# Diagonal term of four attention pairs in the weight stage: from three VectorE passes over row copies to one turned product and six narrow TensorE products

## The reference, cut to what matters

```python
for t in range(S):
    kt, vt, rt, wt = (k[:, :, t], v[:, :, t], r[:, :, t], w[:, :, t])
    cur = np.einsum('bhd,bhe->bhde', u[None] * kt, vt)
    y[:, :, t] = np.einsum('bhd,bhde->bhe', rt, state + cur)
    state = wt[:, :, :, None] * state + np.einsum('bhd,bhe->bhde', kt, vt)
...
a = x @ w1
b = x @ w2
h = a * b @ w3
return (h @ w_out)
```

## Time and profile before

| | us |
|---|---|
| median of 3 runs (lowest, highest) | 981.27 (980.72, 982.27) |
| time of the profiled execution | 980.96 |
| its span, first to last instruction | 979.2 |

### The profile page before, as it was taken

The page is one execution under the profiler, slowest core; times in us unless marked ns, Lnnn a source line. Parts: engine busy times, 40 slices in busy tenths (PEclk is TensorE's granted clock), DMA queues, the critical chain, the costliest instruction groups (busy, mean ns, idle before and its releaser), DMA issues.

```text
span 979.2 us, 18038 instructions
## 1 busy us (share of the span) xinstructions
PE 947.8 (97%) x6825; PEld 894.3 (91%) x6825; DVE 676.2 (69%) x1133; ACT 528.0 (54%) x986; POOL 222.8 (23%) x209
## 2 busy tenths in 40 slices
PE   6989999999999999999989999999999999999995
PEld 4656999999999999999989999999999999999995
DVE  6997769888888875437766765757767468565570
ACT  4454445454555544326545665756657467565560
POOL 0000000202020111021453233333243332334321
PEclk9999999999999999999999999999999999999998
DMA  9996343544445121126557887877968779787751
GB/s 346 302 320 184 115 142 116 160 150 129 134 143 163 50 71 38 51 67 234 188 161 191 237 278 233 250 235 220 307 205 247 254 207 292 218 242 256 200 156 17
DMA packets 94347, 183.74 MB, mean 188 GB/s; under 512 B 18274, under 2 KB 49764, under 8 KB 94260
## 3 DMA queue, kind: packets, MB, share of 16 engines
q1 hardware_dynamic: 80884, 161.90, 50.8%
q0 software_dynamic: 12976, 20.66, 10.2%
q10 hardware_dynamic: 400, 0.02, 0.0%
HBM read 156.94 MB, written 26.97 MB: 188 GB/s over the span
## 4 chain that ended last, share of the span: by engine, by line
PE 87%; DVE 5%; ACT 3%; issue 2%; DMA 1%; SPq 0%; another core or an unknown queue 0%; POOL 0%; DVEq 0%; ACTq 0%; POOLq 0%
PE pp L1231 20%; PE bank L1215 20%; PE bank L786 13%; PE bank L803 7%; PE fx L786 6%; PE fx L803 4%; PE yu L1274 3%; PE pp L184 3%; PE tr L1196 2%; PE yu L1256 1%; PE fx L1256 1%; PE yu L205 1%; PE yu L235 1%; PE tr L193 1%; DVE kdiv L263 1%
## 5 line engine op out<-in xcount | busy, mean ns | idle before, releaser
L1125 POOL DMA_INDIRECT result<-x2s,who x55 | 92.5, 1681 | 290.3 <-ACT x2s L1348 277.4
L1335 DVE SCALAR_TENSOR_TENSOR abl<-bank,abh 128x512 fp32r<-128x512 f32 x96 | 66.2, 691 | 113.7 <-ACT abh L1330 97.5
L976 POOL DMA_INDIRECT slot_entry<-entry,slot_i x48 | 52.1, 1086 | 334.7 <-DVE token_f L965 322.5
L1215 PE MATMUL bank<-xh,set_up_h 128*128 128x256 f32 x384 | 109.2, 284 | 0.0
L1215 PE MATMUL bank<-xh,set_up_l 128*128 128x256 f32 x384 | 108.6, 283 | 0.0
L1215 PE MATMUL bank<-xl,set_up_h 128*128 128x256 f32 x384 | 108.6, 283 | 0.0
L1330 ACT ACTIVATE abh<-bank 128x512 fp32r<-128x512 f32 x96 | 57.5, 599 | 85.1 <-PE bank L1215 79.6
L786 PE MATMUL bank<-xh,w12h 128*128 128x384 f32 x264 | 89.5, 339 | 1.0 <-DVE xl L483 0.9
L786 PE MATMUL bank<-xh,w12l 128*128 128x384 f32 x264 | 88.4, 335 | 0.0
L786 PE MATMUL bank<-xl,w12h 128*128 128x384 f32 x264 | 88.2, 334 | 0.0
L1231 PE MATMUL pp<-set_down_h,abh 128*128 128x384 f32 x256 | 87.7, 342 | 0.0
(11 more groups left out here) (254 smaller groups left out, 2641.4 us busy)
## 6 DMA issues: line engine op xcount, KB each, us to landing
up_raw<-in_moe_w SPq DMA_DIRECT2D x93, 512.0 KB
down_raw<-in_moe_w SPq DMA_DIRECT2D x124, 384.0 KB
wt<-in_w SPq DMA_DIRECT2D x16, 384.0 KB, 3.2
kt<-in_k SPq DMA_DIRECT2D x16, 384.0 KB, 3.1
rt<-in_r SPq DMA_DIRECT2D x16, 384.0 KB, 3.6
vs<-in_v_rows SPq DMA_DIRECT2D x16, 384.0 KB, 3.7
kn<-in_k_rows SPq DMA_DIRECT2D x16, 288.0 KB, 3.2
rn<-in_r_rows SPq DMA_DIRECT2D x16, 288.0 KB, 3.6
```

The lines of the kernel that those rows point to most:

```text
L976: nc.gpsimd.indirect_dma_start(slot_entry, bass.IndirectOffsetOnAxis(slot_i[:, s, n:n + 1], 0), entry[:, s, n, :], None).then_inc(scattere ...
L1125: nc.gpsimd.indirect_dma_start(out, bass.IndirectOffsetOnAxis(who[v % 4][:, s, 0:1], 0), yo[v % 2][:, s, 0:DM], None, bounds_check=N - 1, ...
L1215: last = nc.tensor.matmul(bank[m % 2][:, f * T2:(f + 1) * T2], wp[:, kk, c:c + P], xp[:, kk, :], start=(n == 0), stop=(n == 3 * KD - 1))
L1335: nc.vector.scalar_tensor_tensor(hl[:, 2 * m:2 * m + 2, :].rearrange("p a t -> p (a t)"), bank[m % 2][:, :], 0.0, hh[:, 2 * m:2 * m + 2, : ...
```

## The change

For the pairs 1 to 4 (`by_matmul`) the row tiles are neither loaded nor used. VectorE makes one product of the turned tiles, `weighed[d, t] = rt[d, t] * u_side[d] * kt[d, t]` (128 x 768, one `scalar_tensor_tensor` with the column q of `u_side` as the scalar), where part 0 stood. Where part 1 stood, TensorE makes for each of the six chunks a product with 128 columns of `weighed` as the stationary operand and the 128 x 2 mask `heads` (one in the partitions of head 0 or head 1) as the moving one; the results are the 12 columns of `bank[0]`. Where part 2 stood, ScalarE copies these 12 columns to `diag`. For pair 0 and for the pairs 5 to 15 the three VectorE passes stay; `ruk` and `added` have one buffer in place of two. `u_side` is one more small load (128 x 4) at the start, `heads` are four memsets. Loads of `kt` and `rt` wait for `weighed` as well, and the first `up` step waits for `diag`.

```diff
+        def by_matmul(g):
+            return 1 <= g <= HP
...
         def sp_input_load(sp, b, q, n):
             g, i = HP * b + q, q % 2
+            if n and by_matmul(g - 2):
+                need(sp, weighed_ready, g - 2)
...
         def sp_rows_load(sp, b, q):
             g, i = HP * b + q, q % 2
-            need(sp, rk_ready, g - 1)
+            if by_matmul(g):
+                return
+            need(sp, rk_ready, max(0, g - HP - 1) if g != HP + 1 else 0)
...
         def dve_products(dve, b, q, part):
-            if part == 0:
+            if by_matmul(g):
+                if part == 0:
+                    for n in (1, 2):
+                        dve.wait_ge(loaded[n][i], 16 * (2 * b + q // 2 + 1))
+                    dve.wait_ge(u_side_loaded, 16)
+                    need(dve, diag_full, g - 1)
+                    nc.vector.scalar_tensor_tensor(weighed[:, :], rt[i][:, :], u_side[:, q:q + 1], kt[i][:, :],
+                                                   ALU.mult, ALU.mult).then_inc(weighed_ready, 1)
...
         def dve_diag(dve, b, q):
             g = HP * b + q
-            dve.wait_ge(ruk_ready, g + 1)
+            if by_matmul(g):
+                return
+            dve.wait_ge(ruk_ready, g - HP + 1 if g else 1)
...
+        def pe_diag(pe, b, q):
+            g = HP * b + q
+            pe.wait_ge(weighed_ready, g)
+            if g == 1:
+                pe.wait_ge(heads_ready, 4)
+            need(pe, diag_ready, g)
+            for c in range(NC):
+                last = nc.tensor.matmul(bank[0][:, 2 * c:2 * c + 2], weighed[:, c * C:(c + 1) * C], heads[:, :], start=True, stop=True)
+            last.then_inc(diag_full, 1)
+
+        def act_diag(act, b, q):
+            g = HP * b + q
+            act.wait_ge(diag_full, g)
+            nc.scalar.copy(diag[:, :, :].rearrange("p c h -> p (c h)"), bank[0][:, 0:2 * NC]).then_inc(diag_ready, 1)
...
+            elif step == "diag" and n == 1 and by_matmul(HP * b + q):
+                pe_diag(pe, b, q)
...
+            elif step == "diag" and n == 2 and by_matmul(HP * b + q):
+                act_diag(act, b, q)
...
+                sp.dma_start(u_side[:, :], u_turned[:, :]).then_inc(u_side_loaded, 16)
...
                     if i == 0:
                         pe.wait_ge(wb_free, 6)
+                        pe.wait_ge(diag_ready, HP + 1)
```

More of the change, by code:

```diff
@@ L55, in stands_alone, with program @@
     pool.sem_inc(waited, 1)
-def program(nc, w_turned, k_turned, r_turned, k_rows, r_rows, v_rows, u, w1, w2, w3_turned, w_out, gate_rows, noise_rows, ew1, ew2_rows, out):
+def program(nc, w_turned, k_turned, r_turned, k_rows, r_rows, v_rows, u, u_turned, w1, w2, w3_turned, w_out, gate_rows, noise_rows, ew1, ew2_rows, out):
     f32, f32r, i32 = mybir.dt.float32, mybir.dt.float32r, mybir.dt.int32
@@ L108, in program @@
         rdec = [asb(f"rdec{i}", [P, S]) for i in range(2)]
-        ruk = [asb(f"ruk{i}", [P, NC, 2, D]) for i in range(2)]
+        ruk = asb("ruk", [P, NC, 2, D])
+        weighed = asb("weighed", [P, S])
+        u_side, heads = asb("u_side", [P, HP]), asb("heads", [P, 2])
         kend_t = asb("kend_t", [P, NC - 1, P])
         att = asb("att", [P, 2, 2, 3, C])
-        added = [asb(f"added{i}", [P, NC - 1, D]) for i in range(2)]
+        added = asb("added", [P, NC - 1, D])
         state = [asb(f"state{i}", [P, NC - 1, HB]) for i in range(2)]
@@ L282, in dve_products @@
             g, i = HP * b + q, q % 2
[L283 removed]
+            if by_matmul(g):
[6 more added lines that the diff above has]
+                                                   ALU.mult, ALU.mult).then_inc(weighed_ready, 1)
+            elif part == 0:
                 for n in range(2):
[L285 to L287 removed]
+                    dve.wait_ge(rows_loaded[n][i], 16 * ((g - 2 - i) // 2 if g else 1))
+                need(dve, diag_ready, g)
+                nc.vector.tensor_tensor(ruk[:, :, :, :], kn[i][:, :, :, :], rn[i][:, :, :, :], ALU.mult).then_inc(rk_ready, 1)
             else:
[L289 removed]
+                dve.wait_ge(rk_ready, g - HP + 1 if g else 1)
                 if isinstance(g, int) and g == 0:
@@ L332, in dve_state @@
                 need(dve, state_step, (NC - 2) * g + c - 1)
-                nc.vector.scalar_tensor_tensor(added[q % 2][:, c, :], added[q % 2][:, c - 1, :], decay[q % 2][:, c - 1, C:C + 1],
-                                               added[q % 2][:, c, :], ALU.mult, ALU.add).then_inc(state_step, 1)
+                nc.vector.scalar_tensor_tensor(added[:, c, :], added[:, c - 1, :], decay[q % 2][:, c - 1, C:C + 1],
+                                               added[:, c, :], ALU.mult, ALU.add).then_inc(state_step, 1)
         def act_products(act, b, q):
@@ L338, in act_products @@
             act.wait_ge(yu_full, 3 * g + 1)
-            nc.scalar.copy(added[q % 2][:, :, :], yu[:, 0:(NC - 1) * D].rearrange("p (c x) -> p c x", c=NC - 1)
+            nc.scalar.copy(added[:, :, :], yu[:, 0:(NC - 1) * D].rearrange("p (c x) -> p c x", c=NC - 1)
                            ).then_inc(yu_free, 1)
@@ L350, in act_state @@
                     act.wait_ge(yu_free, g + 1)
-                nc.scalar.activation(state[q % 2][:, c, 0:D], added[q % 2][:, c, :], ACT.Copy,
+                nc.scalar.activation(state[q % 2][:, c, 0:D], added[:, c, :], ACT.Copy,
                                      scale=decay[q % 2][:, c, C:C + 1]).then_inc(state_ready, 1)
@@ L615, in first_dve @@
                 nc.vector.memset(taken[:, :, :], 0.0)
+                for at in range(2):
+                    for h in range(2):
+                        nc.vector.memset(heads[at * HB:(at + 1) * HB, h:h + 1], float(at == h)).then_inc(heads_ready, 1)
                 for i in range(2):
@@ L1692, in rows @@
         return np.pad(x, [(0, 0)] * 5 + [(0, pad)])
+    turned_u = np.pad(a["u"].reshape(HP, 2, D), [(0, 0), (0, 0), (0, HB - D)]).reshape(HP, 2 * HB).T
     return {
         "w": turned(a["w"], 1), "k": turned(a["k"], 0), "r": turned(a["r"], 0),
-        "k_rows": rows(a["k"], 0), "r_rows": rows(a["r"], 0), "v_rows": rows(a["v"], HB - D), "u": a["u"],
+        "k_rows": rows(a["k"], 0), "r_rows": rows(a["r"], 0), "v_rows": rows(a["v"], HB - D), "u": a["u"], "u_turned": turned_u,
         "moe_w1": a["moe_w1"], "moe_w2": a["moe_w2"],
```

11 lines of the change are left out of this document (4 added, 7 removed).

## The result

| | before | changed |
|---|---|---|
| median of 17 runs each, us (lowest, highest) | 982.09 (980.43, 984.49) | 985.59 (983.85, 989.42) |
| ratio (95% interval) | | 1.0035 (1.0024 to 1.0046) |
| profiled execution, us | 980.96 | 983.92 |

The forecast was 980.1 us, range 978.0 to 982.2. The time is outside it, on the slow side, and by the bound of 0.2% the change made the kernel slower, an outcome that had been given 0.04.

The account below looks back on a forecast made before the run. TensorE bounds the kernel, its weight stage being a relay with VectorE. Profiled 980.96 us, plus 0.83 for the four cycles (+1.34 - 1.28 - 0.41 + 1.18), minus 1.69 for the clock, gave 980.1 us, range 978.0 to 982.2.

Parts of the forecast that it names:

- What bounds the kernel: Weight stage as a relay: VectorE last in cycles 2 and 3, TensorE last, or nearly, in cycles 1 and 4.
- m: Added TensorE time per pair for twelve narrow-product records at 0.112 us each: 1.34 us, bounds 0.47 and 1.7.
- the estimate of 0.30 us: Alternative narrow-product price per pair from the skill's 25 ns per record; it would give 977.2 us.
- Cycles 2, 3 and 4: From pair 1's state products to the first `up`, split at pair 2's and 3's scores: -1.28, -0.41, +1.18 us.
- Cycle 1: Stretch up to pair 1's scores: TensorE is last, `weighed` is hidden, so m counts in full, +1.34 us.
- The fall at 22: Granted clock drop at 22 us, after a 1.07 us wait; forecast to stay, being ahead of everything that changes.
- the +0.83 of the prediction: Sum of the four cycles of the weight stage, before any clock effect: +0.83 us, a little slower.
- Transfers give nothing on the path: Eight row copies left out gain 0, since no TensorE wait in cycles 1 to 4 was ended by a transfer.
- The clock, -1.69: The drop to 1.2 GHz at about 72 us, behind a 1.67 us wait, would vanish: -1.69 us.
- both falls go: Rival: earlier `u_all` also removes the clock drop at 22 us, giving 978.4 us; chance 0.12.
- the fall stays, or comes elsewhere: Rival: a slow-clock stretch of about 1.7 us remains behind pair 0, giving 981.8 us; chance 0.22.
- m or `weighed` being large: Rival: with m = 1.7 TensorE is last in every cycle; with a low stretch left, 983.2 us; chance 0.05.

Follow-up runs that it names:

- e2: Kernel before with one `added` buffer and a spacer, so `abh` and later tiles lie where the changed kernel has them: 980.74 us, 1.0033 of the kernel before.
- e11: Kernel before with only the 1.5 MB store to `slot_entry` issued one pair later: 978.65 us, 1.0003 of the kernel before.
- e5: Changed kernel with the turned product for pairs 2 and 3 only, old operand places, `u_side` loaded later: 978.81 us, 0.9974 of the kernel before.
- e6: Changed kernel, four pairs, with old operand places and `u_side` loaded behind pair 1's tiles: 983.66 us, 1.0016 of the kernel before.
- e7: Changed kernel as it is, run again for comparison on the second chip: 985.34 us, 1.0040 of the kernel before.
- e3: Kernel before with six unused narrow products added at each of the change's four places, VectorE passes kept: 976.50 us, 0.9993 of the kernel before.
- e9: Changed kernel, four pairs, with old operand places, `u_side` later and the `slot_entry` store one pair later: 976.52 us, 0.9989 of the kernel before.

## Why the prediction was wrong

**What bounds the kernel.** Right. Every wait behind pair 0 that was named went as said, and the cycles were ended by the engines that were named, with one exception (cycle 1, below).

**The price of the narrow products.** Right: 1.36 us a pair against m = 1.34, at all four places. The row of the routing with the same 128-column stationary operand was the one to trust. That the load of this operand is what is left wasn't tested; the scores, with 128 stationary columns on 48 partitions, take 0.073 us a record (37.19 - 36.32 over 12), so its columns alone don't set the price. The Trainium skill ("TensorE: Matmul & The Clock Gate", section "Back-to-back issue gap") gives the 25 ns, from which the estimate of 0.30 us came, for an isolated gap, and says there that this leaves out the loads of the stationary operand. The measurement decides, 0.113 us a record.

**Cycles 2, 3 and 4.** Right to 0.02 us. From scores to scores: cycle 2 takes 52.88 - 36.32 = 16.56 us against 52.78 - 34.96 = 17.82 before, -1.26 (forecast -1.28). Cycle 3: 17.90 against 18.29, -0.39 (-0.41). Cycle 4: from pair 3's scores to the first `up`, 22.13 us against 22.63 - 1.69 (the fall) = 20.94, +1.19 (+1.18).

**Cycle 1.** The forecast was +1.34, read off a trace in which the products at 21 to 26 us had run at 1.2 GHz. That made TensorE last there and made it ask for `weighed` only at 28.05. Without that fall, VectorE is last before: in the trace of e2, the kernel before with new places, pair 1's scores come 34.35 - 19.12 = 15.23 us behind pair 0's last, with a wait of 1.10 us, against 34.96 - 19.27 = 15.69 in the earlier trace rows. The fall at 22 had cost 0.46. In the change it is 36.32 - 19.79 = 16.53, +1.30: TensorE stands 1.06 us for `weighed`, pays 1.36, and no longer meets the 1.10 for VectorE (together 1.32). The number +1.34 was met by luck: a wait for `weighed` that had been put at 0 and a wait for VectorE that the slow clock had hidden cancel. The wait of 1.06 us stands in all five traces with four pairs. So the sum of the four cycles is +1.30 - 1.26 - 0.39 + 1.19 = +0.84, against the +0.83 of the prediction. The kernel before without falls has its first `up` at 93.70 - 1.69 - 0.46 = 91.55, and the change at 91.55 + 0.84 + 0.52 (`u_all` later) = 92.91, as measured. The forecast for this point, 92.8, was met, but by two errors that cancel: the fall at 22 did not stay (-0.46), and the time of `u_all` did not stay (+0.52). The risk had been noted, that `weighed` has little room in cycle 1; missed was that the room itself came from the slow clock.

**"Transfers give nothing on the path."** Wrong as a rule, since it was read off the waits of before. When the relay is faster, TensorE can come to wait for the block of `w3`: 0 us in the first trace of the change, but 1.76 in its second and 1.83 and 2.44 with the old places. With the store moved the two-pair kernel took 2.0 us less, 0.8 of it this wait by the trace. The sum had no term for it.

**The clock, -1.69.** This step failed too. The stretches at 22 and at 72 were gone in the profiled run, as in the rival "both falls go", though `u_all` came later there and not earlier. But one came at 503, and over the runs the changed kernel has as much of them as before: mean granted clock 0.9925 on either set of its runs, 0.9926 to 0.9930 before. So the gain of -1.69 didn't exist in the median, and the rival "the fall stays, or comes elsewhere", with 981.8 us, was the true one for the clock. A single trace shows one case of something that differs from run to run: behind the wait of 2.53 us, where the earlier trace rows have no fall, the same code has one that begins at 54.6 us, 1.5 us behind this wait, in the trace of e2, and one that begins at 52.4, still within it, in that of e11.

**Everything behind the first `up`.** This is the step that put the time outside the range. The sum has no term for it: it was put at nothing, without a reason given, though the change resizes buffers that lie ahead of the operands used there. It lost 3.75 us in the profiled run: some 2.2 by the even growth, from the shift by 128 bytes, and 1.6 from the fall at 503. The sum of the rival, 981.8, with 2.3 added is 984.1, and the profiled execution took 983.92. In the medians, +0.84 of the stage and 2.3 of the places make 3.1 of the 3.5 us; the rest is within the interval, and a wait for `w3` in some of the runs may be in it.

**Rivals.** None had the places of the operands. Slower by over 0.2% had been given only to m or `weighed` being large, and neither was.

**What stays open.** Where the clock falls in a given run, and why the same gap is followed by a fall in one run and not in another; the gap of 1.9 us at about 500 stands in the traces of before, the change, e5, e6 and e7 and in none from the first and third chip, and a fall follows it in the three with four pairs and not in the two others; why `u_all` is used at anything from 14.6 to 15.6 us (one trace with the small load moved away has 14.77, another 15.52, there behind a wait of 0.99 us for `rn`); and how much of the good times of e3 and e9 is clock to better than a microsecond, since no run could hold it fixed.

## What to carry to other kernels

When a diff adds, drops or resizes a buffer, compare the start addresses of the operands of the most numerous matrix products modulo 256 bytes before and after; a spacer of 128 unused bytes undid the loss here, 2.3 us. Replace a pass by work on another engine only in the cycles in which the first engine was last: at an equal clock the change gains for two pairs of four and loses for all four. Before a wait is priced, ask whether the trace's slow clock made it, and look up which transfer is next late once the relay is faster.

## What the runs showed of the hardware

- **The start of the stationary operand against the moving one changes the rate of products.** 128x128 by 384 columns in fp32r: 173.3 ns at 0, 32, 96 and 192 bytes, 174.7 at 64, 176.2 to 176.8 at 128, 160 and 224, repeating each 256 bytes (but for 174.3 at 256), with TensorE alone. That the distance counts, and not the one address, is shown by the products with `wah` and `wal`, whose four values moved on by two places with the shift of 128 bytes. The Trainium skill ("SBUF — State Buffer", section "Operand start alignment") tells which starts are legal and says of its runs that they "timed nothing"; here they are timed, and differ by up to 2%.
- **A stretch of products with two moving columns** costs 0.113 us a record with a stationary operand of 128 partitions and 128 columns, from start to start (28.07 to 29.43 over 12). The products with 64 stationary and 48 moving columns (L216, 56.66 to 57.38 over 20) cost 0.036; the 0.040 of the prediction is their recorded length.
- **Work that fills a wait can pay by the clock.** Narrow products without any use, put into the kernel before, came with a mean granted clock of 0.9954 against 0.9930 (10 of 11 runs at 0.995 or more, against 4 of 23) and left the time where it was, 0.9993 [0.9984, 1.0002].
